# Windowed attention ahead of two expert layers: key spans copied unscaled, refills ahead of stores, one averaging group per head pair, and TensorE's stages one unit closer behind the scores

## The chip, the cores and the metric

The kernel runs on one core of one Trainium2 chip. The metric is the device time of one execution in microseconds. The kernel before has a median of 1250.22 us over 3 runs (1250.11 to 1251.17).

## The reference

The program computes an attention layer and two layers of experts. The change touches the attention alone; its core is

```
k_sum = k.reshape(B, H, nb, block, D).max(axis=3)
v_sum = v.reshape(B, H, nb, block, D).mean(axis=3)
scores_l = scale * np.matmul(q, k.transpose(0, 1, 3, 2))
mask_l = np.abs(pos[:, None] - pos[None, :]) < window
scores_s = scale * np.einsum('bhsd,bhnd->bhsn', q, k_sum)
scores_s = scores_s + np.log(block)
scores_l_m = np.where(mask_l, scores_l, -1000000000.0)
a = softmax over concatenate([scores_l_m, scores_s])
attn_out = np.matmul(a, np.concatenate([v, v_sum], axis=2))
```

with B = 4 batches, H = 8 heads, S = 768 positions, D = 64, block 32 (so 24 blocks), window 16 and scale 1/8. All is float32. The rows of the result then go through a first expert layer with a gate (argmax over logits, one of 8 experts) and a second with a capacity per expert, assigned in the order of the logits.

## The kernel before

**Tiling.** Two heads make a head pair, so each batch has 4 pairs and the program 16. A pair's 768 queries are worked off in 3 units of 256 queries; a batch has 12 units, the program 48. For 64 queries at a time the window touches a span of 96 keys, so one score matmul is 64 queries against 96 span keys and 24 block maxima, 120 columns. The tile `k_bias` (two buffers, by pair) holds these columns: span keys and maxima in partitions 0 to 63, mask and bias in partitions 64 to 127, met by an identity in the lower half of `q_eye`. So one matmul gives the masked scores.

**Who does what.** For each pair GpSimd (`key_spans`, L471 and L472) multiplies the raw keys `k_raw` by the scale into the 12 overlapping spans of both heads, four instructions. VectorE (`block_maxima`, L1017 and L1020) takes the block maxima of the raw keys in two halves and writes them, scaled, beside the spans. TensorE averages the values per block (`means`, L616), 12 matmuls of 64 columns for each of the two heads; VectorE takes them out of PSUM (L1029), and GpSimd spreads them into `va` (`spread_means`, L482).

**Units.** TensorE, ScalarE and VectorE each run one loop over units n = 0 to 47 and on. In iteration n TensorE does the scores of unit n (L597), the transposes of the probabilities of unit n-2 (L606), at two of three iterations one head of `means` for the next pair, the values of unit n-3 (L634), the transposes of the finished rows of unit n-4 (L648) and, for a batch's last three units, the gate's logits of unit n-5 (L657). ScalarE copies the transposed probabilities out (L867), then the transposed rows (L872), and then does the exponentials of unit n (L859). VectorE takes the maxima of the scores of unit n (L1054), the means, then normalises unit n-3 (L1061 to L1068), and then reduces block maxima of the next pair. The first 6 iterations (`LEAD`) stand ahead of a loop over the batches. After each batch's loop VectorE and ScalarE do the gate's decision (`route`), whose end is `x_ready`.

**Order of the work.** All of it is written by hand; each engine's queue is in order and semaphores join them. SyncE's queue issues all loads and stores of the attention, pair by pair: for pair hp it refills the keys and queries two pairs ahead (`refill_k`, `refill_q`), then the values of the next batch, which wait for `pv_done` of this pair, then stores the rows of pair hp-1. At hp = 0 that store is the last pair's of the batch before, and it waits for `x_ready`. Keys and queries have two buffers, the values four.

Of the kernel before, what the change touches and what calls it, by code (L numbers as in the profile page):

```python
# [15 lines left out]
P = 128  # L16
# [38 lines left out]
LEAD = 6  # L55
# [47 lines left out]
def two_layers_of_experts(nc, q, k, v_win, modality_id, w_gate, modality_bias, w1, w2,  # L103
                          w_gate2, w1b, w2b, out):
    ctx = ExitStack()
    with ctx:
# [57 lines left out]
        ksum_done = sem("ksum_done")  # L164
# [4 lines left out]
        scores_done = sem("scores_done")  # L169
        nmax_done = sem("nmax_done")  # L170
# [158 lines left out]
        def attention_steps(eng, unit, route=None):  # L329
# [5 lines left out]
            def element(b, own):  # L335
                for n in range(LEAD, UNITS + LEAD):
                    unit(b, n, own)
                if route:
                    route(b)
# [8 lines left out]
        def _(sp):  # L348
# [21 lines left out]
            with sp.Fori(0, B) as b:  # L370
                for hp in range(HP):
                    def refill_k(nb, nhp):
                        sp.wait_ge(spans_done, HP * b + hp + 1)
                        sp.wait_ge(ksum_done, HP * b + hp + 1)
                        load_k(nb, nhp)
# [25 lines left out]
                    else:  # L401
# [39 lines left out]
        def _(pool):  # L441
# [4 lines left out]
            pool.dma_start(mid[:, :, :], modality_id.bitcast(I32).rearrange("(j p t) -> p j t", p=P, t=2)).then_inc(modality_loaded, 16)  # L446
            for t in kraw:
                chain(g.memset(t[:, :, 0:WINDOW], 0.0))
                chain(g.memset(t[:, :, WINDOW + S:KW], 0.0))
            g.nop().then_inc(pads_ready, 1)  # L450
            chain(g.memset(ident[:, :], 0.0))
            chain(g.affine_select(out=ident[:, :], in_=ident[:, :], compare_op=ALU.not_equal, fill=1.0,
                                  base=0, pattern=[[-1, P]], channel_multiplier=1))
            g.nop().then_inc(eye_ready, 1)
            span = span_mask[D:P, 0:WK]
            chain(g.memset(span_mask[D:P, WK:PW], math.log(BLOCK)))
# [5 lines left out]
            g.nop().then_inc(mask_ready, 1)  # L462

            def key_spans(m):
# [3 lines left out]
                for h in range(2):  # L468
                    pieces = kraw[m % 2][:, h, 0:S].rearrange("d (j c) -> d j c", c=QB)
                    after = kraw[m % 2][:, h, QB:QB + S].rearrange("d (j c) -> d j c", c=QB)  # L470
                    g.tensor_scalar(kbt[m % 2][0:D, h, :, 0:QB], pieces, SCALE, None, ALU.mult).then_inc(pool_chain, 1)  # L471
                    last = g.tensor_scalar(kbt[m % 2][0:D, h, :, QB:WK], after[:, :, 0:WK - QB], SCALE, None, ALU.mult)  # L472
                    last.then_inc(pool_chain, 1)
                    chain.n += 2
                pool.wait_ge(pool_chain, chain.n)
                g.nop().then_inc(spans_done, 1)  # L476

            def spread_means(m):
                pool.wait_ge(means_taken, 2 * (m + 1))
# [5 lines left out]
            key_spans(0)  # L485
# [97 lines left out]
        def _(pe):  # L583
            mm, tr = nc.tensor.matmul, nc.tensor.transpose
            def scores(b, n):
                hp, i = n // PU, n % PU
                if i == 0:
                    pe.wait_ge(q_loaded[hp % 2], 16 * (HP // 2 * b + hp // 2 + 1))
                    pe.wait_ge(spans_done, HP * b + hp + 1)
                    pe.wait_ge(ksum_done, HP * b + hp + 1)  # L590
# [18 lines left out]
            def means(b, m, h, n):  # L609
                pe.wait_ge(vw_loaded[m % HP], 16 * (b + m // HP + 1))  # L610
                if m or h or not isinstance(b, int):
                    pe.wait_ge(means_taken, 2 * (HP * b + m) + h)
                if n >= 5:
                    pe.wait_ge(x_done, UNITS * b + n - 4)
                for j in range(NQ):
                    last = mm(bank[4 + (n + 1) % 2][WK:PW, MEAN0:MEAN0 + D], average[:, j, :], va[m % HP][0:WK, h, j, 0:D],  # L616
# [3 lines left out]
            def values(b, n):  # L620
# [7 lines left out]
                else:  # L628
                    pe.wait_ge(means_taken, 4)
# [31 lines left out]
            pe.wait_ge(const_ready, 1)  # L661
# [3 lines left out]
            def unit(b, n, own):  # L665

                own(scores, n, n)
                if n >= 2:
# [10 lines left out]
                if n >= 5:  # L679
                    own(first_logits, n - 5, n - 5)  # L680

            means(0, 0, 0, 0)
            means(0, 0, 1, 1)
# [161 lines left out]
        def _(act):  # L845
# [3 lines left out]
            for t in qe:  # L849
                last = nc.scalar.activation(t[D:P, :, :].rearrange("p h (j u) -> p (h j) u", u=QB),  # L850
                                            ident[D:P, D:P].unsqueeze(1).to_broadcast([P - D, 2 * NQ, QB]), ACT.Copy)
            last.then_inc(eye_rows, 1)

            def exponentials(b, n):
# [27 lines left out]
            def unit(b, n, own):  # L882

                if n >= 2:
                    own(copy_probs, n - 2, n - 2)
                if n >= 4:
                    own(copy_x, n - 4, n - 4)
                own(exponentials, n, n)
                if n >= 5:
                    own(copy_logits, n - 5, n - 5)  # L890
# [5 lines left out]
            attention_steps(act, unit, route)  # L896
# [101 lines left out]
        def _(dve):  # L998
# [4 lines left out]
            for t in kbt:  # L1003
# [4 lines left out]
            vec.nop().then_inc(bias_rows, 1)  # L1008

            def block_maxima(b, m, h):  # L1010

                if h == 0:
                    dve.wait_ge(k_loaded[m % 2], 16 * (HP // 2 * b + m // 2 + 1))
                    if m or not isinstance(b, int):
                        dve.wait_ge(ksum_done, HP * b + m)
                own_keys = kraw[m % 2][:, h, WINDOW:WINDOW + S].rearrange("p (n t) -> p n t", t=BLOCK)
                vec.tensor_reduce(ksum[:, h, :], own_keys, AXX, ALU.max).then_inc(bmax_done, 1)  # L1017
                if h == 1:
                    dve.wait_ge(bmax_done, 2 * (HP * b + m) + 2)
                    vec.tensor_scalar(kbt[m % 2][0:D, :, :, WK:PW], ksum[:, :, :].unsqueeze(2).to_broadcast([D, 2, NQ, NB]), SCALE, None, ALU.mult  # L1020
# [432 lines left out]
```

## Time and profile before

| | |
|---|---|
| median of 3 runs | 1250.22 us |
| the profiled execution | 1257.53 us |
| its span | 1255.8 us, mean granted clock 0.84 |
| first score matmul | 24.76 us from the span's start |
| scores of the last unit (47) | 257.43 us |
| first weights of the experts requested | 276.85 us |
| TensorE matmuls busy | 956.8 us (76%) |
| VectorE, ScalarE, GpSimd busy | 560.7, 325.4, 281.2 us |

Times in views are microseconds from the span's start. In a timeline a row is one instruction or a run of equal ones: start, duration, engine and line, what it writes and reads, and in square brackets how long the engine was idle before and what ended that. PE is TensorE's matmuls and PEld its weight loads, DVE is VectorE, ACT ScalarE, POOL GpSimd, SP SyncE; a q behind a name is that engine's queue. A float32 matmul shows as two records, so 8 matmuls are x16. The end of a matmul row is modelled, so the distance from one row's start to the next one's is what a stage takes.

### The profile page before, as it was taken

Reading aid. Unit: us, or ns where it says so; the run is one execution under the profiler, and the core shown is the slowest. Engines: PE = TensorE matmul, PEld = TensorE weight load, DVE = VectorE, ACT = ScalarE, POOL = GpSimd, SP = SyncE. Lnnn points to the kernel's source line nnn. Section 1 sums busy time; section 2 is a strip of 40 time slices with the busy share of each in tenths; the row PEclk is TensorE's granted clock in tenths of the full one; section 3 lists DMA queues with packets and bytes.
Section 4 is the critical chain, followed back from the end, with each engine's and each line's share of the span. In section 5 each row is a group of like instructions: output and inputs, shape, how many; then the busy total and the mean of one; then the engine's idle time right before and its main releaser. Section 6 shows DMA issues by size and latency. Waiting matters only on the chain.

```text
span 1255.8 us, 24355 instructions
## 1 busy us (share of the span) xinstructions
PE 956.8 (76%) x7844; PEld 792.0 (63%) x7845; DVE 560.7 (45%) x1581; ACT 325.4 (26%) x659; POOL 281.2 (22%) x324
## 2 busy tenths in 40 slices
PE   3898988872799999999994333333229999999995
PEld 3676777661588888888883222222227888888884
DVE  3645444547422222222223776667663434444431
ACT  2443434322322222222223000000004443443421
POOL 7755535501012111211111000000001222222220
PEclk9997878865899999999997555555559999999998
DMA  7565536424611111111112000000023343444310
GB/s 142 116 122 115 113 86 119 85 49 165 241 42 42 42 34 34 44 41 34 35 41 84 5 0 0 0 0 0 0 77 108 115 171 126 159 176 176 109 34 25
DMA packets 45988, 97.49 MB, mean 78 GB/s; under 512 B 7248, under 2 KB 19584, under 8 KB 45952
## 3 DMA queue, kind: packets, MB, share of 16 engines
q1 hardware_dynamic: 37888, 70.56, 20.9%
q0 software_dynamic: 8064, 26.46, 6.2%
q8 instruction: 21, 0.34, 0.1%
q14 instruction: 15, 0.12, 0.0%
HBM read 77.49 MB, written 19.51 MB: 77 GB/s over the span
## 4 chain that ended last, share of the span: by engine, by line
PE 59%; issue 24%; POOL 5%; DVE 5%; DMA 4%; ACT 1%; SPq 1%; DVEq 0%; ACTq 0%; POOLq 0%
PE bank L704 41%; DMA k_raw<-in_k 3%; PE bank L728 3%; PE bank L616 3%; PE bank L597 3%; POOL k_bias L471 3%; PE bank L711 2%; PE bank L657 2%; PE bank L751 2%; PE bank L606 1%; PE bank L634 1%; POOL k_bias L472 1%; PE bank L744 1%; PE bank L648 1%; DMA xg<-x_rows,gidx 1%
## 5 line engine op out<-in xcount | busy, mean ns | idle before, releaser
L704 PE MATMUL bank<-W,xh 128*128 (+1 forms) x784 | 254.8, 407 | 13.5 <-DVE gates L1202 10.6
L704 PE MATMUL bank<-W,hh 128*128 (+1 forms) x784 | 252.5, 403 | 10.2 <-DVE hl L1209 10.2
L704 PEld LDWEIGHTS bank<-W,xh 128*128 128x128 f32 x784 | 146.4, 192 | 46.3 <-issue 11.3
L704 PEld LDWEIGHTS bank<-W,hh 128*128 128x128 f32 x784 | 145.3, 190 | 42.5 <-issue 9.0
L704 PE MATMUL bank<-W,xl 128*128 (+1 forms) x392 | 156.5, 399 | 0.0
L704 PE MATMUL bank<-W,hl 128*128 (+1 forms) x392 | 156.0, 398 | 0.0
L795 PE MATMUL bank<-ge,cb 128*8 128x16 bf16 x1344 | 42.3, 172 | 106.5 <-DVE ge L1321 106.5
L538 POOL COPY sidx<-idx 128x1 int32 (+1 forms) x49 | 27.2, 556 | 366.9 <-DVE y L1217 247.7
L795 PEld LDWEIGHTS bank<-ge,cb 128*8 128x8 bf16 x1344 | 36.1, 83 | 111.8 <-DVE ge L1321 111.8
L1209 DVE TENSOR_TENSOR hl<-bank,hh 128x512 fp32r<-128x512 f32 x98 | 63.1, 686 | 95.9 <-ACT hh L898 91.7
L529 POOL COPY gidx<-idx 128x1 int32 (+1 forms) x50 | 10.6, 212 | 406.3 <-DVEq L1152 293.1
L898 ACT ACTIVATE xh<-bank 128x512 fp32r<-128x512 f32 x50 | 29.8, 595 | 269.5 <-PE bank L711 269.5
L1196 DVE TENSOR_TENSOR W<-raw_w,W 128x1024 f32 (+1 forms) x80 | 93.0, 1218 | 6.1 <-ACT W L898 5.9
L471 POOL TENSOR_SCALAR k_bias<-k_raw 64x768 f32<-64x768 f32 x32 | 70.2, 2195 | 92.5 <-DMA k_raw<-in_k 91.8
L898 ACT ACTIVATE hh<-bank 128x512 fp32r<-128x512 f32 x98 | 53.1, 597 | 137.1 <-PE bank L728 137.1
L704 PEld LDWEIGHTS bank<-W,xl 128*128 128x128 f32 x392 | 74.9, 191 | 18.2
L898 ACT ACTIVATE W<-raw_w 128x1024 f32 (+1 forms) x80 | 78.6, 1055 | 29.7 <-SPq L424 28.0
L704 PEld LDWEIGHTS bank<-W,hl 128*128 128x128 f32 x392 | 74.3, 190 | 17.8
L922 ACT ACTIVATE hid<-bank 128x512 f32<-128x512 f32 x98 | 59.1, 604 | 86.9 <-PE bank L704 86.9
L597 PE MATMUL bank<-k_bias,q_eye 128*64 128x120 f32 x768 | 59.1, 305 | 23.5 <-POOLq L476 21.4
L616 PE MATMUL bank<-va,average 96*24 96x64 f32 x768 | 59.1, 243 | 19.3 <-POOLq L496 18.9
L1200 DVE TENSOR_TENSOR xl<-bank,xh 128x512 fp32r<-128x512 f32 x50 | 34.6, 692 | 82.7 <-ACT xh L898 82.7
(234 smaller groups left out, 1289.5 us busy)
## 6 DMA issues: line engine op xcount, KB each, us to landing
raw_w<-in_moe_w SPq DMA_DIRECT2D x20, 2048.0 KB, 9.4
va<-in_v_win SPq DMA_DIRECT2D x16, 585.0 KB, 4.9
k_raw<-in_k SPq DMA_DIRECT2D x16, 384.0 KB, 8.1
q_eye<-in_q SPq DMA_DIRECT2D x16, 384.0 KB, 8.1
x_rows<-x SPq DMA_DIRECT2D x12, 384.0 KB, 9.2
x_rows<-x SPq DMA_DIRECT2D x4, 387.0 KB, 5.4
xg<-x_rows,gidx POOLq DMA_INDIRECT x26, 3.4
y_rows<-y,sidx POOLq DMA_INDIRECT x25, 2.8
```

Of the source, the lines that this page charges most:

```text
L471: g.tensor_scalar(kbt[m % 2][0:D, h, :, 0:QB], pieces, SCALE, None, ALU.mult).then_inc(pool_chain, 1)
L538: chain(g.tensor_copy(sidx[:, :], idx[:, bass.ds(val(i), 1)]))
L597: last = mm(bank[n % 2][QB * s_:QB * s_ + QB, PW * (2 * t + h):PW * (2 * t + h) + PW], qe[hp % 2][:, h, QB * j:QB * j + QB], kbt[hp % 2][: ...
L616: last = mm(bank[4 + (n + 1) % 2][WK:PW, MEAN0:MEAN0 + D], average[:, j, :], va[m % HP][0:WK, h, j, 0:D], start=j == 0, stop=j == NQ - 1)
L704: last = mm(ps, lhs[a][:, c, :], rhs[b](c), start=c == 0 and t == 0, stop=c == n - 1 and t == 2)
L728: last = tr(bank[2 + c // 4][:, P * (c % 4):P * (c % 4) + P], hid[:, P * c:P * c + P], ident[:, :])
L795: last = mm(bank[7][0:E, 0:KSEARCH], cb[:, j, :], ge[:, j, :], start=j == 0, stop=j == TC - 1)
L898: copy = lambda o, a: nc.scalar.activation(o, a, ACT.Copy)
L922: nc.scalar.activation(hid[:, 512 * half:512 * half + 512], bank[half][:, :], ACT.Relu).then_inc(relu_done[st], 1)
L1196: tt(o, r, hi.bitcast(F32), ALU.subtract).then_inc(wlo_done[st], 1)
L1200: ins = tt(xl[:, :, :].rearrange("p c t -> p (c t)"), bank[4][:, :], xh[:, :, :].rearrange("p c t -> p (c t)").bitcast(F32), ALU.subtract)
L1209: tt(hl[:, f, :].rearrange("p c t -> p (c t)"), bank[2 + half][:, :], hh[:, f, :].rearrange("p c t -> p (c t)").bitcast(F32), ALU.subtract ...
```

## The change

- `LEAD` is 5: TensorE does the transposes of the probabilities of unit n-1 in iteration n, values of unit n-2, transposed rows of n-3, logits of n-4; ScalarE and VectorE follow.
- GpSimd copies the keys into the spans unscaled, four `tensor_copy`, and in a fifth copies the block maxima, which VectorE wrote before; it waits for VectorE's two reductions. `ksum_done` is gone. The scale is applied after the scores: ScalarE's exponential gets `scale=SCALE`, and VectorE multiplies the 4 negated maxima of a unit by it, a new instruction of 128x4 behind a wait on the reduction. The bias of the block columns is divided by the scale.
- SyncE's store that waits for `x_ready` stands at hp = 1, behind that pair's refills and its other store.
- `means` of a pair is one group of 12 matmuls of 128 columns (both heads), in every third iteration, and VectorE takes it out in one copy.
- At the start GpSimd's span mask comes first and the load of the modality last; VectorE builds the spans of the first pair (`first_spans`); TensorE does the first scores ahead of the first means.
- `route` is cut in two: its first three VectorE instructions follow the iteration in which the last logits come.

```diff
-LEAD = 6
+LEAD = 5
...
-                    else:
+                    if hp == 1:
                         with sp.If(b > 0):
                             sp.wait_ge(x_ready, b)
...
-                    g.tensor_scalar(kbt[m % 2][0:D, h, :, 0:QB], pieces, SCALE, None, ALU.mult).then_inc(pool_chain, 1)
-                    last = g.tensor_scalar(kbt[m % 2][0:D, h, :, QB:WK], after[:, :, 0:WK - QB], SCALE, None, ALU.mult)
...
+                    chain(g.tensor_copy(kbt[m % 2][0:D, h, :, 0:QB], pieces))
+                    chain(g.tensor_copy(kbt[m % 2][0:D, h, :, QB:WK], later[:, :, 0:WK - QB]))
+                pool.wait_ge(bmax_done, 2 * (m + 1))
+                chain(g.tensor_copy(kbt[m % 2][0:D, :, :, WK:PW], ksum[:, :, :].unsqueeze(2).to_broadcast([D, 2, NQ, NB])))
                 g.nop().then_inc(spans_done, 1)
...
-                if n >= 2:
-                    own(transpose_probs, n - 2, n - 2)
-                if n % PU < 2:
-                    m = n // PU + 1
-                    own(means, PU * m, m, n % PU, n)
-                if n >= 3:
-                    own(values, n - 3, n - 3)
-                if n >= 4:
-                    own(transpose_rows, n - 4, n - 4)
...
+                if n >= 1:
+                    own(transpose_probs, n - 1, n - 1)
...
+                if n % PU == 1:
+                    m = n // PU + 1
+                    own(means, PU * m, m, n)
+                if n >= 2:
+                    own(values, n - 2, n - 2)
+                if n >= 3:
+                    own(transpose_rows, n - 3, n - 3)
...
-                                                bias=nmax[n % 2][:, a:a + 1])
+                                                bias=nmax[n % 2][:, a:a + 1], scale=SCALE)
...
-                                  AXX, ALU.max, negate=True).then_inc(nmax_done, 1)
+                                  AXX, ALU.max, negate=True).then_inc(max_done, 1)
+                dve.wait_ge(max_done, UNITS * b + n + 1)
+                vec.tensor_scalar(nmax[n % 2][:, :], nmax[n % 2][:, :], SCALE, None, ALU.mult).then_inc(nmax_done, 1)
```

TensorE's queue, iteration 7 of the first batch. Of the buffer numbers, a unit's scores are in bank 0 or 1, its transposed probabilities in bank 2 or 3, its values in bank 4 or 5 and its rows in bank 6 or 7, by the unit's parity; `probs` goes round three buffers. Before:

```order
L597 MATMUL bank1<-k_bias0,q_eye0 64x120 x8
L606 MATMUL bank3<-ident,probs2 120x128 x4
L612 REGISTER_ALU
L616 MATMUL bank4<-va3,average 24x64 x12
L634 MATMUL bank4<-va1,pt0 64x65 x8
L648 MATMUL bank7<-ident,x 128x128 x2
```

and of the changed kernel:

```order
L596 MATMUL bank1<-k_bias0,q_eye0 64x120 x8
L601 REGISTER_ALU
L605 MATMUL bank2<-ident,probs0 120x128 x4
L609 ISA
L615 MATMUL bank5<-va3,average 24x128 x12
L633 MATMUL bank5<-va1,pt1 64x65 x8
L647 MATMUL bank6<-ident,x 128x128 x2
```

The stages stand in the same order, but behind the scores of unit 7 the transposes now read `probs0`, the exponentials of unit 6, where they read `probs2`, those of unit 5. ScalarE's queue for iteration 6 reads before

```order
L867 ACTIVATE pt0<-bank2 120x512
L872 ACTIVATE xt<-bank6 128x256
L855 REGISTER_ALU
L857 REGISTER_ALU
L859 ACTIVATE probs0<-bank0,nmax0 128x120 x4
```

and of the changed kernel

```order
L864 REGISTER_ALU
L865 ACTIVATE pt1<-bank3 120x512
L870 ACTIVATE xt<-bank7 128x256
L853 REGISTER_ALU
L857 ACTIVATE probs0<-bank0,nmax0 128x120 x4
```

The copies belong to units 5 and 3 now, before to 4 and 2; the exponentials of unit 6 still stand behind the copy of the transposed rows, which TensorE makes last in its iteration 6. In SyncE's queue the store that waits for `x_ready` (129 columns wide) moves like this:

```order
-L402 COMPARE_AND_BRANCH
-L396 ISA
-L396 DMA x_rows<-x 128x6x129
-L402 UNCONDITIONAL_BRANCH
+L387 UNCONDITIONAL_BRANCH
 L373 REGISTER_ALU
 L353 ISA
 L353 DMA k_raw<-in_k 64x2x768
```

The load of the keys of a batch's last pair no longer stands behind it; the store now comes one pair later, ahead of the load of the next batch's first keys.

## Rows read from the trace of the kernel before

**Rows 1.** The chain that ended last, 24.8 to 276.8 us, by line:
```profile
by line: DMA k_raw<-in_k 16.6%; PE bank L597 13.3%; PE bank L616 12.4%; POOL k_bias L471 10.0%; PE bank L657 8.5%; PE bank L606 7.2%; PE bank L634 7.1%; POOL k_bias L472 5.4%; issue 3.8%; PE bank L648 3.5%; SPq L396 1.2%; DVE ksum L1017 1.1
```
**Rows 2.** Busy time by stretch: length; PE, PEld, DVE, ACT, POOL; granted clock; DMA share, GB/s:
```profile
71.70:132.50 60.80, 54.26 (x698) 45.79 (x698) 30.76 (x76) 23.88 (x72) 33.49 (x21) 0.86 0.56 114
132.50:202.70 70.20, 61.86 (x698) 52.65 (x698) 30.62 (x80) 24.77 (x76) 31.82 (x20) 0.76 0.51 101
...
276.80:1255.80 979.00, 732.62 (x5060) 602.13 (x5060) 430.17 (x1252) 222.05 (x351) 139.44 (x198) 0.83 0.21 70
32.00:34.00 2.00, 1.19 (x19) 0.87 (x17) 1.49 (x2) 1.05 (x3) 1.60 (x4) 1.00 0.46 104
```
**Rows 3.** Pieces of that chain in order of time: start, duration, what:
```profile
55.59 9.41 DMA k_raw<-in_k
...
70.43 1.15 POOL k_bias L472
71.74 1.87 PE bank L597 x16
...
83.72 1.69 PE bank L657 x16
...
150.16 2.69 PE bank L616 x24
```
**Rows 4.** Who waited for whom, 0 to 210 us: total, times, longest:
```profile
POOL k_bias L471 <- DMA k_raw<-in_k: 67.4, 10, 16.4
```
**Rows 5.** Timeline, one iteration with `means` at the full clock:
```profile
77.11 1.04 PE L597 MATMUL bank<-k_bias,q_eye 128*64 128x120 f32 x16
...
78.08 0.65 PE L606 MATMUL bank<-ident,probs 128*120 128x128 f32 x4
...
78.66 1.53 PE L616 MATMUL bank<-va,average 96*24 96x64 f32 x24
...
80.12 0.69 PE L634 MATMUL bank<-va,pt 120*64 120x65 f32 x16
...
80.74 0.44 PE L648 MATMUL bank<-ident,x 128*128 128x128 f32 x2
...
81.11 1.04 PE L597 MATMUL bank<-k_bias,q_eye 128*64 128x120 f32 x16
...
81.22 0.39 ACT L872 ACTIVATE xt<-bank 128x256 f32<-128x256 f32 x1 [1.85 <-PE bank L648]
...
81.50 1.11 ACT L859 ACTIVATE probs<-bank,nmax 128x120 f32<-128x120 f32 x4
...
81.92 0.93 DVE L1017 TENSOR_REDUCE ksum<-k_raw 64x24 f32<-64x768 f32 x1
```
**Rows 6.** GpSimd's groups by form: busy, mean ns of one | idle before, releaser:
```profile
L471 POOL TENSOR_SCALAR k_bias<-k_raw 64x768 f32<-64x768 f32 x32 | 70.2, 2195 | 92.5 <-DMA k_raw<-in_k 91.8 <-POOL iota_e L510 0.3 <-POOL span_mask L460 0.2
...
L482 POOL COPY va<-vst 24x1536 f32<-24x1536 f32 x16 | 23.4, 1465 | 11.3 <-DVE vst L1029 8.2 <-POOL k_bias L472 3.1
```
**Rows 7.** Timeline of the start and of two later places:
```profile
6.50 4.40 POOL L471 TENSOR_SCALAR k_bias<-k_raw 64x768 f32<-64x768 f32 x1 [0.21 <-POOL span_mask L460]
...
33.08 1.04 PE L597 MATMUL bank<-k_bias,q_eye 128*64 128x120 f32 x16 [0.81 <-DVE k_bias L1020]
...
43.00 1.43 DVE L1041 CAST midf<-mid 128x24 f32<-128x24 int32 x1
...
99.15 0.35 SPq L357 DMA_DIRECT2D va<-in_v_win  x1
...
104.07 0.43 SPq L396 DMA_DIRECT2D x_rows<-x  x1
...
257.43 1.04 PE L597 MATMUL bank<-k_bias,q_eye 128*64 128x120 f32 x16
```
**Rows 8.** DMA issues: KB each, median us to landing (first: the load issued at 8.75):
```profile
va<-in_v_win SPq DMA_DIRECT2D x1, 585.0 KB, 9.7
```
**Rows 9.** The same view over the whole span:
```profile
k_raw<-in_k SPq DMA_DIRECT2D x16, 384.0 KB, 8.1
```

More of the change, by code:

```diff
@@ L337, in element @@
                     unit(b, n, own)
-                if route:
-                    route(b)
+                    if route and n in route:
+                        route[n](b)
             with eng.Fori(0, B - 1) as b:
@@ L445, in _ @@
                 pool.sem_inc(stored, 16)
[L446 to L454, printed above, removed]
             span = span_mask[D:P, 0:WK]
-            chain(g.memset(span_mask[D:P, WK:PW], math.log(BLOCK)))
+            chain(g.memset(span_mask[D:P, WK:PW], math.log(BLOCK) / SCALE))
             chain(g.memset(span, 0.0))
@@ L462, in _ @@
             g.nop().then_inc(mask_ready, 1)
+            chain(g.memset(ident[:, :], 0.0))
+            chain(g.affine_select(out=ident[:, :], in_=ident[:, :], compare_op=ALU.not_equal, fill=1.0,
+                                  base=0, pattern=[[-1, P]], channel_multiplier=1))
+            g.nop().then_inc(eye_ready, 1)
+            for t in kraw:
+                chain(g.memset(t[:, :, 0:WINDOW], 0.0))
+                chain(g.memset(t[:, :, WINDOW + S:KW], 0.0))
+            g.nop().then_inc(pads_ready, 1)
+            pool.dma_start(mid[:, :, :], modality_id.bitcast(I32).rearrange("(j p t) -> p j t", p=P, t=2)).then_inc(modality_loaded, 16)
             def key_spans(m):
@@ L607, in transpose_probs, with means @@
                 last.then_inc(pt_done, 1)
-            def means(b, m, h, n):
+            def means(b, m, n):
                 pe.wait_ge(vw_loaded[m % HP], 16 * (b + m // HP + 1))
[L611 to L614, printed above, removed]
+                if m or not isinstance(b, int):
+                    pe.wait_ge(means_taken, HP * b + m)
+                if n >= 4:
+                    pe.wait_ge(x_done, UNITS * b + n - 3)
                 for j in range(NQ):
-                    last = mm(bank[4 + (n + 1) % 2][WK:PW, MEAN0:MEAN0 + D], average[:, j, :], va[m % HP][0:WK, h, j, 0:D],
+                    last = mm(bank[4 + n % 2][WK:PW, MEAN0:MEAN0 + 2 * D], average[:, j, :], va[m % HP][0:WK, :, j, 0:D],
                               start=j == 0, stop=j == NQ - 1)
@@ L882, in unit @@
             def unit(b, n, own):
-                if n >= 2:
-                    own(copy_probs, n - 2, n - 2)
+                if n >= 1:
+                    own(copy_probs, n - 1, n - 1)
+                if n >= 3:
+                    own(copy_x, n - 3, n - 3)
+                own(exponentials, n, n)
                 if n >= 4:
[L887 to L890, printed above, removed]
+                    own(copy_logits, n - 4, n - 4)
             def route(b):
@@ L894, in route @@
                 nc.scalar.activation(lexp[:, :, :], lsh[:, :, :], ACT.Exp).then_inc(route_exp_out, 1)
-            attention_steps(act, unit, route)
+            attention_steps(act, unit, {UNITS + LEAD - 1: route})
             copy = lambda o, a: nc.scalar.activation(o, a, ACT.Copy)
@@ L1083, in unit, with route_shift @@
                     token_biases()
[L1085 removed]
+            def route_shift(b):
                 chain.start(pre + per * b)
@@ L1103, in route @@
                 assert chain.n == per, (chain.n, per)
-            attention_steps(dve, unit, route)
+            attention_steps(dve, unit, {UNITS + LEAD - 2: route_shift, UNITS + LEAD - 1: route})
             tt, ts, stt, red = vec.tensor_tensor, vec.tensor_scalar, vec.scalar_tensor_tensor, vec.tensor_reduce
```

80 lines of the change are left out of this document (43 added, 37 removed).

## The prediction, made before the changed kernel ran

> **What bounds the kernel now.** I read the chain of waits first. Over the whole span the experts' matmuls lead it, and nothing of them changes, so the question is the attention, 24.8 to 276.8 us. There the chain is not TensorE alone: 16.6% of it is the load of the keys, 15.4% GpSimd's making of the spans out of them [rows 1]. The busy table by stretch says the same from the other side: in 60.8 us, the second batch's length, TensorE works 54.3 us at a granted clock of 0.86, in the third batch, 70.2 us long, 61.9 us at 0.76 [rows 2]. So it loses both ways, by standing and by the low clock afterwards. The chain in order of time shows one such stand: keys asked for at 55.59 land 9.41 us later, GpSimd's last span ends at 71.58, and the scores start at 71.74 in 1.87 us instead of 1.04 [rows 3, 5]. GpSimd waited 67.4 us in 10 such places [rows 4].
>
> The timeline at the full clock gives what TensorE needs. From one start to the next: scores 0.97, transposes 0.58, one head of means 1.46, values 0.62, transposed rows 0.37, together 4.00 [rows 5]; without means 2.54; the gate's logits add 1.69 [rows 3].
>
> **The change, part by part.** I count in iterations, with t(n) the start of the scores of unit n.
>
> *Keys.* The next load of keys goes out 1.3 us after the values of a pair's last unit. Those come one iteration earlier now, so the keys of a pair have the whole of four iterations less 1.3 us: from t(3p-4)+1.3 to t(3p). Landing takes 8.1 us in the median and 9.41 in the example [rows 3, 9]. GpSimd's multiplies take 2195 ns for 768 elements, 2.86 ns each; its only plain copy takes 1465 ns for 1536, 0.95 ns each [rows 6]. At the copy's rate the four copies cost 2 x (0.73+0.37) plus starts, about 2.9 us instead of 6.6, and the fifth, of the maxima, 0.64. The bounds are a copy like the copy (3.5 us in all) and a copy like the multiply (6.6 + 1.6 = 8.2 us). I take the first, since it is the same operation, though on 24 partitions there and 64 here.
>
> The GPSIMD Engine Reference of the Trainium skill (section 3.1, on elementwise cycle accounting) speaks against this: it gives one rate, about a cycle per element, for bodies of at most two operations, so a multiply by a constant and a copy would cost the same and the copies would bring nothing. The rows disagree, 2.86 ns against 0.95 [rows 6]; by the page's rule this would be the case of slow copies below, 1280.
>
> So keys landing at t(3p-4)+9.4 to 10.7 are spans by +14.2 at the latest. Four iterations are 15.4 (below). The second half of the maxima is made behind the normalising of the iteration before t(3p-1) and ends 1.74 us into an iteration (81.92+0.93-81.11) [rows 5]; with the fifth copy the spans are ready about 2.7 us into one that lasts 3.1. The load is hidden, narrowly.
>
> *The exponentials.* Here the closer stages cost. ScalarE does the exponentials of unit n behind the copy of transposed rows that TensorE makes last in its iteration n, before as after. They start at t(n+1)+0.39 and end at +1.50 (81.50+1.11-81.11) [rows 5]. Before, their transposes came two iterations later. Now they come at t(n+1)+0.97, so TensorE waits until about +1.57: 0.6 us in every iteration, unless logits stand between (three of twelve). A plain iteration is then 3.14, one with means 0.6 above its work.
>
> *Means.* 12 matmuls of 128 columns replace 24 of 64. The 24 records of 64 columns take 1.46 us at the full clock and 2.69 at the low one [rows 3, 5], 61 and 112 ns each, so they follow the array's clock, and 64 columns at two cycles are 53 ns of the 61. With 128 I take 115 ns, 2.75 us a group against 2.92 for both before. The bounds: 61 ns (1.46 us) if the 61 were fixed, and 145 ns (0.58/4, transposes of 128 columns) [rows 5], 3.48 us.
>
> *Route.* SyncE issued the values at 99.15 and the store behind `x_ready` at 104.07 [rows 7]: 4.9 us for the keys behind it, three times; gone. In its place the two stores at hp = 1 put 384 KB more ahead of the next keys in one iteration of two batches; at the 185 GB/s that 1.74 MB in 9.41 us make, 2.1 us, of which about 1.5 shows, since VectorE's block maxima stand in its queue ahead of the maxima of the scores. The second half of `route` holds the maxima of unit 5 to about 4.8 us into its iteration, where the exponentials would start at 3.5: 1.2 us a batch.
>
> *A batch.* 8 plain iterations of 2.54, 4 with means of 5.29, three logits of 1.69, nine waits of 0.6, 1.2 for route: 20.3+21.2+5.1+5.4+1.2 = 53.2 us. Before, the second and third batch took 60.8 and 70.2 [rows 2], and all three after the first 62.9 on average (257.43-71.74, and one iteration of 3.1) [rows 3, 7].
>
> *Small edits.* The 128x4 multiply on VectorE, some 0.25 us a unit, lies before exponentials that wait for TensorE anyhow; if that cover goes it is 0.25 a unit, 12 us in all. The scale in the activation I take as free, since its activations already carry a bias.
>
> *Start.* The first scores no longer stand behind GpSimd's first spans, but the values of unit 0 need both first means and the second pair's maxima: the values of pair 1 land at 8.75+9.7 = 18.45 [rows 8], its means take some 4 us while the clock is low, then 0.23+0.94 on VectorE and 0.64+1.47 on GpSimd, about 25.9, so scores of unit 3 at about 27 instead of 33.08 [rows 7]. VectorE's wide copies slow GpSimd at the start (4.40 us for a multiply of 2.2) [rows 6, 7]; the same load hides that. From unit 3 to 12: six plain 3.14, three with means 5.9, and 2.0 for the modality's instructions on VectorE (from 43.00 on) [rows 7]: 38.6, so unit 12 at 65.6 instead of 71.74.
>
> *Sum.* The scores of unit 47: 65.6 + 3 x 53.2 - 3.14 = 222.1, plus 3.0 for the two double stores. Six gaps of 2 to 3 us stay (modality, three routes, two double stores); each may bring the low clock for a few stages (2.69 for 1.46), 1.5 us each, 9 in all. So 234.1 instead of 257.43 [rows 7]: 23.3 earlier. The drain behind it is one iteration shorter, 2.0. Together 25.3. The 979 us behind it [rows 2] only move. The profiled execution took 1257.5, 7.3 above the median, so it would be 1232, and the median 1250.2-25.3 = 1225.
>
> **Rivals.**
> *Means cheap*: 61 ns a record. For it: scores of 120 columns also show 0.97 us for 16, 61 each. Against: those alternate between two halves of the array's columns and can overlap. 16 x 1.29 = 21 us more gained: 1204.
> *Keys still late*: the loads are packed into 12.2 us a pair instead of 15.5, and if they land after 10.7 or more, VectorE's block maxima hold everything behind them. Nine pairs at about 1.2 and nearly as much for the clock: some 17 us given back, 1242. For it: 9.41 [rows 3] is not rare; against: the DMA share is only 0.51 to 0.56 [rows 2].
> *GpSimd copies as slowly as it multiplies* (slower than before): 8.2 us from landing to spans, so scores 18.9 us after t(3p-4), 3.5 late. It decides from about 4.8 us on. Three pairs a batch give 3 x (3.5+2.5 for the clock) = 18 us; with 53.2 that is 71.2 against 62.9 before, 25 over three batches, and two such pairs in the first put unit 12 at 77.6, 6 late. About 30 slower: 1280.
> *The small waits bring the low clock down for good*: TensorE waits 0.6 us in three of four iterations. For it: after a stand of 2 us at 71.74 the scores went at the low clock [rows 3]. At that clock the stages take 1.85 times as long (2.69 for 1.46), some 86 us a batch instead of 53: about 1355. The Trainium skill has such a case ("TensorE: Matmul & The Clock Gate", section on a second HAM failure mode): an engine that idles briefly between groups can fall back and recover over and over. Against it: from 32 to 34 us TensorE worked 1.19 of 2.0 us and was granted 1.00 [rows 2].
>
> **How the numbers follow.** The forecast (keys hidden, exponentials set the pace) has 0.60, its own range 1214 to 1236. Means cheap 0.14, keys late 0.16, slow copies 0.05, low clock 0.03, the rest 0.02. The range reaches from 1203, the cheap means, to 1242, the late keys; outside lie the two slower cases and tails. A measurement of this kernel tells a change from none at about 0.2%, 2.5 us. Faster by more: all but the slow cases and a tail of the late keys, 0.91; within it 0.02; slower 0.07.
>
> **What would show it.** Right: scores to scores about 3.1 us in plain iterations, each with TensorE released by ScalarE's exponentials; GpSimd copies of 0.7 to 0.9 us; a means group of 2.7 to 2.8; keys landed before VectorE's queue reaches them; clock near 1 between 70 and 230. Wrong: plain iterations of 2.5 (the exponentials did not wait), GpSimd releasing TensorE at pair starts (keys or copies late), a means group of 1.5, or the expert stages changing their length.

## The result: slower where faster was forecast, and the profile after

The changed kernel takes 1261.86 us (median of 4 runs, 1258.05 to 1267.49); the kernel before took 1250.26 beside it (4 runs). The ratio is 1.0091, with a 95% interval of 1.0055 to 1.0127: 0.9% slower, and 37 us over the forecast of 1225. The profiled executions are 1259.62 (span 1257.4) and 1257.53 (span 1255.8), only 2 us apart, because the profiled execution of before was a long one for that kernel.

The experts' stage has kept its length: 978.63 us behind the first request for weights, which went out at 278.77 (979.00 behind 276.8 before [rows 2]). So it is again the attention alone. Its chain by line from the first scores (10.94) on:

```profile
by line: DMA k_raw<-in_k 20.4%; PE bank L615 13.2%; PE bank L605 9.1%; PE bank L633 8.9%; PE bank L656 7.5%; ACT probs L857 7.2%; PE bank L596 6.4%; issue 5.9%; PE bank L647 4.4%; DVE nmax L1061 2.0%; DVE ksum L1016 1.8%; DVE oh L326 1.8%; 
```

GpSimd's spans, 15.4% of the chain before [rows 1], are gone from it, as was meant. The keys have not gone: 20.4% where 16.6% stood. The busy table by stretch (length; PE, PEld, DVE, ACT, POOL; granted clock; DMA share, GB/s) has the second and third batch first, and then two stretches inside the second:

```profile
68.37:137.66 69.29, 51.27 (x600) 41.72 (x600) 32.61 (x85) 24.65 (x76) 19.96 (x25) 0.87 0.69 115
137.66:202.85 65.19, 50.90 (x601) 41.47 (x600) 32.37 (x84) 24.72 (x76) 19.08 (x25) 0.89 0.65 107
...
120.00:125.00 5.00, 4.49 (x58) 3.66 (x55) 0.00 (x0) 0.82 (x2) 0.00 (x0) 1.00 1.29 95
278.77:1257.40 978.63, 732.81 (x5060) 602.44 (x5060) 430.18 (x1252) 222.02 (x351) 139.17 (x198) 0.83 0.21 70
```

A batch takes 69.3 and 65.2 us where 53.2 was forecast. TensorE's work did shrink (51 busy us for 54.3 and 61.9), and its clock is no worse than before (0.87 and 0.89 for 0.86 and 0.76 [rows 2]); it stands 18 and 14 us a batch. And there is something odd from 120 to 125 us: the DMA engines are counted busier than in any stretch of [rows 2] (1.29; the packets' times overlap), yet they move 95 GB/s, less than the 114 at a share of 0.56 in [rows 2]. What lies there is a pair of stores. From the timeline and the chain of that place:

```profile
111.27 0.33 SPq L357 DMA_DIRECT2D va<-in_v_win  x1
111.79 1.15 SPq L395 DMA_DIRECT2D x_rows<-x  x2
113.28 0.95 SPq L353 DMA_DIRECT2D k_raw<-in_k  x1
...
131.42 0.94 DVE L1016 TENSOR_REDUCE ksum<-k_raw 64x24 f32<-64x768 f32 x1 [13.24 <-DMA k_raw<-in_k]
...
133.77 1.11 ACT L857 ACTIVATE probs<-bank,nmax 128x120 f32<-128x120 f32 x4 [9.83 <-DVE nmax L1064]
...
134.94 1.11 PE L605 MATMUL bank<-ident,probs 128*120 128x128 f32 x4 [10.45 <-ACT probs L857]
```

```profile
113.28 18.11 DMA k_raw<-in_k
181.22 15.38 DMA k_raw<-in_k
```

The keys asked for right behind the two stores land after 18.11 us, against 9.41 in [rows 3]. VectorE's block maxima wait for them with the maxima of the scores behind them in the queue, so ScalarE gets no maxima and TensorE no probabilities: it stands 10.45 us, although the scores whose probabilities it waits for (unit 22, at 117.60) were made before and need none of the late keys. The iteration from unit 23 to 24 takes 14.2 us instead of 3.1, the one a batch later (35 to 36) 11.5. The issue view over the span says the same of medians (KB each, us to landing):

```profile
k_raw<-in_k SPq DMA_DIRECT2D x16, 384.0 KB, 9.9
...
x_rows<-x SPq DMA_DIRECT2D x12, 384.0 KB, 10.8
x_rows<-x SPq DMA_DIRECT2D x4, 387.0 KB, 12.5
```

The keys took 8.1 before [rows 9]; the store of 387 KB, which now stands behind another, is the slowest of all.

The second new gap is at the gate's decision, once a batch; the timeline from unit 17 on:

```profile
94.11 1.04 PE L596 MATMUL bank<-k_bias,q_eye 128*64 128x120 f32 x16
...
96.95 1.47 POOL L480 COPY va<-vst 24x1536 f32<-24x1536 f32 x1 [0.23 <-POOL k_bias L473]
97.15 1.49 DVE L326 TENSOR_TENSOR oh<-iota_e,lidx 128x48 f32 x1
97.30 1.04 PE L596 MATMUL bank<-k_bias,q_eye 128*64 128x120 f32 x16
...
100.27 0.66 DVE L1061 TENSOR_REDUCE nmax<-bank 128x4 f32<-128x480 f32 x1 [0.76 <-DVE x L1115]
...
101.63 1.11 ACT L857 ACTIVATE probs<-bank,nmax 128x120 f32<-128x120 f32 x4 [3.84 <-DVE nmax L1064]
...
102.80 1.11 PE L605 MATMUL bank<-ident,probs 128*120 128x128 f32 x4 [4.46 <-ACT probs L857]
```

The scores of unit 17 start at 94.11 and those of unit 18 at 97.30. The maxima of unit 17 start only at 100.27, behind the second half of `route`, and its exponentials at 101.63, so TensorE stands 4.46 us ahead of its transposes in iteration 18 and then goes at the lower clock (transposes in 1.11 us instead of 0.65). These three iterations take 8.2, 7.5 and 8.3 us instead of 3.1.

What came as forecast is in these rows, a plain iteration (unit 46 to 47), the groups of GpSimd and `means` (busy, mean ns of one | idle before), and the list of waits:

```profile
253.84 0.65 PE L605 MATMUL bank<-ident,probs 128*120 128x128 f32 x4 [0.51 <-ACT probs L857]
254.42 0.69 PE L633 MATMUL bank<-va,pt 120*64 120x65 f32 x16
255.03 0.44 PE L647 MATMUL bank<-ident,x 128*128 128x128 f32 x2
255.40 1.04 PE L596 MATMUL bank<-k_bias,q_eye 128*64 128x120 f32 x16
```

```profile
L615 PE MATMUL bank<-va,average 96*24 96x128 f32 x384 | 47.2, 280 | 0.6 <-POOLq L493 0.6
...
L470 POOL COPY k_bias<-k_raw 64x768 f32<-64x768 f32 x30 | 24.6, 820 | 69.1 <-DMA k_raw<-in_k 67.3 <-POOL va L480 0.5 <-POOL iota_e L507 0.2
...
L471 POOL COPY k_bias<-k_raw 64x384 f32<-64x384 f32 x30 | 15.1, 502 | 1.8
```

```profile
POOL k_bias L473 <- DVE ksum L1016: 81.7, 15, 12.8
POOL k_bias L470 <- DMA k_raw<-in_k: 67.3, 10, 15.7
...
PE bank L605 <- ACT probs L857: 48.2, 31, 10.4
```

In iteration 46 TensorE waits 0.51 us for the exponentials and the iteration is 3.1 us long; the copies take 820 ns instead of the 2195 of [rows 6]. The records of L615 overlap, so their mean is no length; from start to start a group of 24 takes 2.73 us (90.40 to 93.13).

### The profile page after: what moved, and what is told of

Same layout as the page of the kernel before. It is cut to its first block, busy times and chain, and to the rows that moved or that the text cites. A ratio compares the mean times of both kernels' runs of the same rounds, so it can differ in the third digit from the quotient of the medians.

```text
span 1257.4 us, 23551 instructions
## 1 busy us (share of the span) xinstructions
PE 945.7 (75%) x7460; PEld 776.0 (62%) x7461; DVE 568.1 (45%) x1602; ACT 325.4 (26%) x659; POOL 227.9 (18%) x335
## 4 chain that ended last, share of the span: by engine, by line
PE 59%; issue 25%; DVE 5%; DMA 5%; ACT 2%; POOL 2%; SPq 1%; DVEq 0%; ACTq 0%; POOLq 0%
PE bank L703 41%; DMA k_raw<-in_k 4%; PE bank L727 3%; PE bank L615 3%; PE bank L605 2%; PE bank L633 2%; PE bank L710 2%; PE bank L656 2%; PE bank L750 2%; ACT probs L857 2%; PE bank L596 1%; PE bank L647 1%; PE bank L743 1%; ACT W L896 1%; DMA xg<-x_rows,gidx 0%
## 5 line engine op out<-in xcount | busy, mean ns | idle before, releaser
L703 PE MATMUL bank<-W,xh 128*128 (+1 forms) x784 | 254.6, 406 | 13.4 <-DVE gates L1216 10.5
L703 PEld LDWEIGHTS bank<-W,xl 128*128 128x128 f32 x392 | 74.9, 191 | 18.1
L605 PE MATMUL bank<-ident,probs 128*120 128x128 f32 x192 | 36.4, 320 | 48.2 <-ACT probs L857 48.2
L896 ACT ACTIVATE yt<-bank 128x512 f32<-128x512 f32 x25 | 14.9, 597 | 217.7 <-PE bank L743 217.7
L1239 DVE TENSOR_SCALAR y<-bank,gates 128x512 f32<-128x512 f32 x25 | 18.8, 751 | 114.6 <-PE bank L703 114.6
```

The costliest lines, as they stand in the source:

```text
L605: last = tr(bank[2 + n % 2][0:PW, P * a:P * a + P], probs[n % 3][:, a, :], ident[:, :])
L703: last = mm(ps, lhs[a][:, c, :], rhs[b](c), start=c == 0 and t == 0, stop=c == n - 1 and t == 2)
L896: copy = lambda o, a: nc.scalar.activation(o, a, ACT.Copy)
```

## The experiments

Theory: the two stores together make the keys late, and that is most of the loss; `route` on VectorE is the rest. Rivals: the volume ahead of the keys (then the shape of rows is indifferent); the refills ahead of the store as such (then separating the two stores at the same hp brings nothing); the copies or the closer stages themselves cost the time. Each run's ratio is to runs of the kernel before on its own chip. "Start of the experts" is the first request for weights, 276.85 before and 278.77 after.

**1. The store back at hp = 0.** In the changed kernel:

```diff
-                    if hp == 1:
+                    if hp == 0:
                         with sp.If(b > 0):
                             sp.wait_ge(x_ready, b)
```

> The changed kernel with one edit undone: the store of a batch's last pair stands at hp = 0 again, where the kernel before had it, alone behind that pair's refills. Theory A (two stores of x_rows in flight at once slow each other and everything queued with them; in the changed kernel keys landed after 18.1 and 15.4 us behind the double store, where they took 8 to 10 elsewhere): no landing of keys above 11 us, rows of 516 bytes at about 32 ns a packet instead of 129, and the time falls by 10 to 18 us, to about 1246. Theory B (the transfers are simply packed closer because every stage is faster): landings of 12 us and more stay, and the time stays within 3 us of the changed kernel's, since the keys now also wait some 5 us for x_ready three times.

Measured: 1238.34 us, ratio 0.990 [0.985, 0.995]. Start of the experts 257.48. The keys' median landing is 8.0 and none after the first three takes over 9.7:

```profile
k_raw<-in_k SPq DMA_DIRECT2D x16, 384.0 KB, 8.0
...
x_rows<-x SPq DMA_DIRECT2D x4, 387.0 KB, 5.5
```

So the placing of one store decides the sign of the whole change: some 24 us, more than the 10 to 18 expected, although the wait for `x_ready` (a store issued 5.8 us behind the values) is back with it.

**2. The move alone.** In the kernel before:

```diff
-                    else:
+                    if hp == 1:
                         with sp.If(b > 0):
                             sp.wait_ge(x_ready, b)
```

> The kernel before with that one edit alone: the store that waits for x_ready moved to hp = 1. Theory A: the two stores meet here too, keys behind them land after 13 us or more twice, and the kernel is 5 to 20 us slower than before. Theory B: the three waits of 4.9 us are gone and no landing grows beyond 11 us: 5 to 12 us faster than before.

Measured: 1247.93 (10 runs), ratio 0.9985 [0.996, 1.001]: no change, so neither of the two times expected came, but the late landings did. The waits for `x_ready` are gone; its chain has

```profile
115.89 16.27 DMA k_raw<-in_k
```

and the iterations at these places take 16.3 and 11.6 us. The slow landing belongs to the move, not to the stages or the copies. That the kernel before pays for it with what the same move gains, and the changed kernel with its closer stages does not, is a reading that no run separates.

**3. Both stores at hp = 1, but apart.** In the changed kernel, the `x_ready` store goes between the queries' refill and the next values:

```diff
                         refill_q(b, hp + 2)
+                    if hp == 1:
+                        with sp.If(b > 0):
+                            sp.wait_ge(x_ready, b)
+                            store_x(..., HP - 1)
                     with sp.If(b < B - 1):
...
                         store_x(b, hp - 1)
-                    if hp == 1:
...
```

> The changed kernel with the store that waits for x_ready at hp = 1 but ahead of that pair's refill of values, so that about 8 us and the values' load lie between the two stores. Theory A: the landings above 13 us go, packets of 516 bytes fall from 129 ns to under 50, and the time falls by 10 to 20 us, to 1242 to 1252. Theory B: as many bytes in as short a stretch, so landings stay and the time is within 3 us of the changed kernel's.

Measured: 1237.22 (7 runs), ratio 0.9904 [0.9875, 0.9933]. Start of the experts 258.04. The store goes out at 97.29, the pair's own at 110.01, and the keys behind it land in 9.31 us:

```profile
97.29 0.43 SPq L386 DMA_DIRECT2D x_rows<-x  x1
...
110.01 0.41 SPq L386 DMA_DIRECT2D x_rows<-x  x1
110.77 0.58 SPq L353 DMA_DIRECT2D k_raw<-in_k  x1
```

```profile
110.77 9.31 DMA k_raw<-in_k
```

The refills ahead of the store were no fault; the wide store (129 columns) right behind the narrow one (128) was. The iteration from unit 23 to 24 is 3.7 us. The experiment changes two things at once, the distance of the two stores and their order: the wide one now goes first. The last batch has no values to refill, so there the same two stores go out 0.81 us apart, wide first. They land as they do alone (5.0 and 9.9 us in the batch shown above), and the wide one's packets take 28.7 ns:

```profile
213.39 1.18 SPq L386 DMA_DIRECT2D x_rows<-x  x2
...
x_rows<-x SPq DMA_DIRECT2D x1, 387.0 KB, 5.4
x_rows<-x SPq DMA_DIRECT2D x1, 384.0 KB, 9.9
```

So closeness alone is not the fault. Whether the order decides or how far the two really overlap, no run tests.

**4. Rows padded, the stores still together.** The rows of `x_rows` are 513 floats, 2052 bytes, apart, so their pieces of 512 bytes begin at any multiple of 4 bytes. Here they are 2112 bytes apart; the last store is 144 columns wide. VectorE fills them and the gathers' tile `xg` is as wide, two edits not shown:

```diff
-XW = DM + 1
+XW = DM + 16
...
-                        cols = slice(P * shp, P * shp + P + (shp == HP - 1))
+                        cols = slice(P * shp, P * shp + P + 16 * (shp == HP - 1))
```

> The changed kernel with rows of x_rows 528 floats apart (2112 bytes, a multiple of 64) instead of 513 (2052 bytes); the last pair's store is then 144 columns wide, 576 bytes a row, and the double store stays. Theory A with misaligned rows as the cause of the slowness: the wide packets fall from 129 ns to about 35, the landings to 10 or 11 us, and the time by 10 to 18 us. Theory A with the mere overlap of two stores as the cause: wide packets stay near 129 ns and the time within 4 us of the changed kernel's. The gathers of the first expert layer get 3% more bytes, which should not show.

Measured: 1237.34, ratio 0.989 [0.983, 0.995]. Start of the experts 259.78; their stage is no shorter (981.0 us). Landings are shorter than in any kernel so far, with more bytes in each fourth store:

```profile
k_raw<-in_k SPq DMA_DIRECT2D x16, 384.0 KB, 6.7
...
x_rows<-x SPq DMA_DIRECT2D x4, 432.0 KB, 4.9
```

That excludes the volume. The rival of the double store's bytes, which is also how the prediction priced it, falls.

**5. The kernel before with padded rows** tells whether the pitch matters where stores are single. It is before with the edit of experiment 4.

> The kernel before with its rows padded to 2112 bytes (144 columns in the last of the four stores instead of 129); its two stores are never in flight together. If misaligned rows cost only where two stores overlap, as the short packets of 31.5 ns in the kernel before and 34.2 ns in the changed kernel with its stores apart suggest, the time is that of the kernel before, 0.995 to 1.003 of it, and the 512-byte packets fall from 50.9 ns to about 31 without anyone waiting for them. If misaligned rows cost in every store, the keys behind the stores land 1 to 2 us earlier and the ratio is 0.985 to 0.993.

Measured: 1250.26 (10 runs), ratio 0.999 [0.996, 1.002], the same; yet the keys land in 6.7 us (median) instead of 8.1, and the one that took 9.41 [rows 3] now takes 6.7. The first half of the expectation holds for the time, the second for the landings: single stores are slowed by the pitch too, but before the change nobody collects those 2.7 us. The records of the packets put the kernels side by side: mean ns of one packet of the narrow stores (512 bytes, all twelve) and of the wide ones (516 or 576 bytes, the first three; the fourth goes out alone behind the last batch, at 32 to 35 ns everywhere):

```
kernel                       row pitch  stores    512 B   516 or 576 B
before                       2052 B     single     50.9     31.5
after                        2052 B     double     58.3    129.0
2, move alone                2052 B     double     52.9     99.4
1, store back                2052 B     single     50.5     31.3
3, apart                     2052 B     single     53.0     34.7
4, padded                    2112 B     double     31.0     33.8
5, before padded             2112 B     single     30.4     31.5
```

It takes both, the odd pitch and a wide store right behind a narrow one, to make a packet of 516 bytes take 99 to 129 ns instead of 31 to 35. "Single" is not quite that in the last batch: the kernel before issues a wide store at 235.87 and a narrow one at 238.24, before the first has landed, and experiment 3 the two above; in both the wide one goes first and its packets take 31.8 and 28.7 ns. Why the other order is slow (two writers in one piece of memory, or something else) no run here shows.

**6. `route` one iteration earlier.** Experiment 3 with the second half of `route` moved up to the first, in both queues:

```diff
-            attention_steps(act, unit, {UNITS + LEAD - 1: route})
+            attention_steps(act, unit, {UNITS + LEAD - 2: route})
...
-            attention_steps(dve, unit, {UNITS + LEAD - 2: route_shift, UNITS + LEAD - 1: route})
+            attention_steps(dve, unit, {UNITS + LEAD - 2: lambda b: (route_shift(b), route(b))})
```

> The version with the stores apart, and the whole of route, on ScalarE and VectorE, one iteration earlier, ahead of the iteration with means that TensorE works 5.3 us on. Theory A (route stands in VectorE's queue ahead of the maxima of unit 5 and costs its iteration 4 to 5 us: 8.2, 7.7 and 8.2 us instead of 3.1, and about 0.8 in the one behind): 12 to 17 us faster, the three iterations 3.1 to 4 us. Theory B (the delay only moves, since route now stands ahead of the maxima of unit 4): the iteration of unit 4 grows from 5.3 to 8 us or more and the time stays within 4 us.

Measured: 1224.80, ratio 0.9778 [0.972, 0.984]. Start of the experts 243.97, 14.1 us earlier than in experiment 3. The iterations that took 8.2, 7.7 and 8.2 us in experiment 3 take 3.1, 3.0 and 3.1, since the iteration in which the decision now lies, one with `means` (5.3 us), is long enough to cover it:

```profile
90.72 0.38 DVE L326 TENSOR_TENSOR oh<-iota_e,lidx 128x48 f32 x1
...
92.65 0.66 DVE L1061 TENSOR_REDUCE nmax<-bank 128x4 f32<-128x480 f32 x1 [0.67 <-DVE x L1115]
```

**7. The same edit with the stores together**, that is the changed kernel with the edit of experiment 6, asks whether the two losses add.

> The changed kernel with the whole of route one iteration earlier on ScalarE and VectorE, and the two stores still together at hp = 1. If the two losses, double store and route, are separate and add, this stands as far below the changed kernel as the same edit did with the stores apart (12 to 16 us): 1246 to 1250, 0.996 to 1.000 of the kernel before. If most of route's delay lies beside the late keys, it brings under 6 us: 1256 to 1261, 1.004 to 1.009.

Measured: 1241.75 (9 runs), ratio 0.9939 [0.991, 0.997]. Against 1.0091 that is 1.5%, some 19 us (the two come from different chips, and the two intervals leave 13 to 25), at or above the 12 to 16 expected. They add, as far as these intervals tell.

**8. The spans multiplied again.** Experiment 3 with the four copies as multiplies by 1.0:

```diff
-                    chain(g.tensor_copy(kbt[m % 2][0:D, h, :, 0:QB], pieces))
+                    chain(g.tensor_scalar(kbt[m % 2][0:D, h, :, 0:QB], pieces, 1.0, None, ALU.mult))
```

> The version with the stores apart, and GpSimd making the four span pieces with a multiply by 1.0 instead of a copy (same values). It prices the copies. Theory A (the copies are a third as long and lie on the path from keys to scores): multiplies of 2.1 and 1.2 us, 4 us more from landing to spans, scores late by 2 us or more at most pairs and the low clock behind it: 15 to 30 us slower than with the copies. Theory B (the landing and VectorE's maxima cover them): within 4 us.

Measured: 1248.36 (10 runs), ratio 0.9963 [0.994, 0.999], so the copies are worth 0.6% or 7 us in this setting, between the two cases expected. Start of the experts 267.54 against 258.04.

```profile
L470 POOL TENSOR_SCALAR k_bias<-k_raw 64x768 f32<-64x768 f32 x30 | 63.7, 2124 | 48.7 <-DMA k_raw<-in_k 39.7 <-PE bank L596 6.9 <-POOL iota_e L507 0.3
```

The same bytes in the same shape: 2124 ns by a multiply, 820 by a copy. The case of slow copies had the direction right and, at some 30 us, was too dear: from unit 23 to 24 it takes 6.1 us instead of 3.7 and the iteration behind it 4.5 instead of 2.9, so 3.9 at this pair, where 6 were counted at each.

**9. Exponentials ahead of the copy of the rows.** Experiment 3 with ScalarE's two last steps exchanged:

```diff
+                own(exponentials, n, n)
...
-                own(exponentials, n, n)
```

> The version with the stores apart (1237 us), and on ScalarE the exponentials of unit n now ahead of the copy of the transposed rows of unit n-3. Theory A (that order makes TensorE wait 0.5 us in nine of twelve iterations, the price of the closer stages): plain iterations fall from 3.1 to 2.5 or 2.7 us, the sum of TensorE's waits for the exponentials from 37.6 to under 15 us, and the time by 8 to 16 us; not by the full 18, since four iterations then last 12.9 us and keys need about 13.3. Theory B (something else, such as the spans at 2.7 us into an iteration or VectorE's work, stands right behind): plain iterations stay at 3.0 or more and the time within 4 us.

Measured: 1232.54, ratio 0.984 [0.978, 0.990], some 8 us under experiment 3 by the ratios, whose intervals overlap. The wait of 0.51 us is gone and plain iterations take 2.7 instead of 3.1 us, but the second and third batch take 58.5 and 57.8 us, as in experiment 3 (58.0 and 57.6), and unit 47 starts at 235.07 instead of 234.67. What the stages save comes back as waits for the keys (from unit 23 to 24 6.0 us instead of 3.7) and at `route` (8.8 instead of 8.2). Only the drain, the stretch behind the last unit's scores, keeps it: start of the experts 17.6 us behind unit 47 instead of 23.4.

**10. All of it:** stores apart, rows padded, exponentials first, `route` early.

> Stores apart, rows of x_rows 2112 bytes apart, exponentials first and route early, together. If each part's gain stands by itself: 1237 less 8 to 16, less 12 to 17, less some 2 for faster landings, so 1202 to 1217. If the transfers of the keys become the bound (1.74 MB a pair in 9 us at best, against iterations that give 10.6 us a pair): waits for the keys come back and the time stays above 1217.

Measured: 1204.05, ratio 0.9638 [0.957, 0.971], 3.6% under the kernel before and the fastest of all. Start of the experts 219.10. Its second and third batch:

```profile
64.85:112.39 47.54, 46.87 (x601) 38.62 (x601) 31.31 (x83) 24.29 (x77) 19.06 (x24) 1.00 0.63 151
112.39:159.91 47.52, 46.86 (x600) 38.60 (x600) 31.70 (x83) 24.27 (x77) 19.07 (x24) 1.00 0.64 152
```

TensorE is busy 46.9 of 47.5 us and is granted 1.00 throughout. Now the padding and the exchange on ScalarE pay: together they bring another 1.4% over experiment 6 (0.5 to 2.3 by the intervals), where the padding changed nothing for the kernel before, and the exchange left the batches as long as they were.

## Why the prediction was wrong

The forecast was 1225 and the time 1261.9. The sum had 1.5 us for the low clock behind each of the two double stores and the three decisions, and those are counted with them here. By the ratios, each taken of 1250, the 37 us are:

| step of the prediction | forecast | measured | missed |
|---|---|---|---|
| two double stores, 3.0 and 3.0 for the clock | 6.0 | after less experiment 3: 0.0187 of 1250 = 23.4 | 17.4 |
| `route`, 1.2 a batch and 4.5 for the clock | 8.1 | experiment 3 less 6: 0.0126 = 15.8 | 7.7 |
| all the rest, gained: 25.3 + 6.0 + 8.1 | 39.4 | 1 less experiment 6: 0.0222 = 27.7 | 11.7 |

The runs come from different chips and each ratio has an interval of 0.3 to 0.6% to either side, so a row is good to some 6 to 8 us. The base (5.4) and the drain (6.0), both below, come to the 11.7 of the last row.

**The double store** is the step that failed. The prediction saw it ("the two stores at hp = 1 put 384 KB more ahead of the next keys") and priced it by bytes over a mean rate, 2.1 us, of which 1.5 shows. It measured 18.1 and 15.4 us of landing where 9.3 is usual, and 11 and 8 us more in the iteration that waits. The error was to take the queue as a pipe of constant rate. In the trace of before these two stores go out 9.6 us apart (104.07 and 113.69), or 2.4 with the wide one first (235.87 and 238.24), and the first lands in 5.4, so it had no row for a wide store right behind a narrow one. The step had one answer, without the two bounds given elsewhere; at the least the far end should have stood beside it, as a rival that ends slower. The rival "keys still late" has the right mechanism (block maxima hold everything behind them) with another cause, and at 1242 it was too cheap.

**`route`** had its mechanism right and its size wrong: 1.2 us a batch against 4.4 to 5.2 in the three iterations. The prediction let the maxima of the next scores come "about 4.8 us into" the iteration. In the trace they start 6.16 us into it (94.11 to 100.27), their scaling ends at 101.60, 7.5 us in, and TensorE then starts at the lower clock. 1.1 us of the 7.5 is one instruction, `oh`, 1.49 us long instead of the 0.38 it takes in experiment 6. It lies beside GpSimd's copy from 96.95 to 98.42, and ends at 98.64.

**The base.** The sum was made against a profiled execution of 1257.5 us and its 25.3 taken off a median of 1250.2. But that execution is 7.3 us over the median, and its third batch took 70.2 us [rows 2]; in experiment 5, the same kernel but for the padding and the same in time, the profiled execution took 1250.84 and its third batch 62.7. So the surplus lies most likely in that batch, in the waits for keys that the change removes. A gain summed against a long execution is too large for a typical one. Experiment 6 shows it: its span is 33.1 us below that of before (1222.7 to 1255.8), its median only some 27.7, so 5.4 of the miss.

**The drain** was to be 2.0 us shorter; from unit 47 to the weights it takes 23.4 us instead of 19.4, so 6.0 were missed. The exponentials of the last units wait for nothing but their own place behind the rows' copy, TensorE stands 1.48 us and then goes at the lower clock. With the exponentials first it takes 17.6.

**Right** were: the plain iteration (3.14 forecast, 3.1) and its wait (0.6, measured 0.51); `means` at 2.73 for 2.75, so not the cheap case; the copies at 0.82 and 0.50 us for 0.73 and 0.37; unit 3 at 26.84 for 27; the keys all but hidden where no double store is in front (3.7 us from unit 23 to 24 in experiment 3, 3.1 in experiment 4). Without the two mis-sized terms the sum up to the last unit holds: a batch of 53.2 less 1.2 for `route` is 52.0, and in experiment 6 the batches take 53.6 and 52.2; unit 47 would be at 234.1 less 3.0, 3.6 and 7.5 for the clock, 220.0, and is at 220.62. The low clock did not take over: 0.87 and 0.89.

The multiply by the scale, "some 0.25 us a unit" beside other work, is mostly that, but not always. Beside GpSimd's copies it takes up to 0.86 us. Its line's instructions (ns, min/median/max), and two neighbours in a timeline:

```profile
L1064 DVE TENSOR_SCALAR nmax<-nmax x48: 170/171/861, 13.8 to 257.2; 128x4 f32<-128x4 f32 x48
```

```profile
73.92 0.82 POOL L470 COPY k_bias<-k_raw 64x768 f32<-64x768 f32 x1
74.00 0.77 DVE L1064 TENSOR_SCALAR nmax<-nmax 128x4 f32<-128x4 f32 x1
```

The multiply ends at 74.77, GpSimd's copy at 74.74. In the place at 131 us it is the same: the multiply from 132.97 ends at 133.74, the copy from 132.89 at 133.71. The Trainium skill says why ("SBUF — State Buffer", section "SBUF: two separate sides"): GpSimd and some instructions of VectorE, those with two SBUF inputs among them, share a pair of ports under an exclusive lock, and the later one waits for the whole of the other's instruction. `oh`, with two inputs, and the scaling, from SBUF to SBUF, behave so. The maxima of the scores, which read PSUM, do not (0.66 us at 100.27 ahead of the copies, 0.64 at 132.29 beside one), nor do those of the keys, which read one input in SBUF (0.94 at 131.42 beside the copy from 131.45). The multiply that the unscaled copies ask of VectorE therefore costs more beside them than the prediction counted.

**Open:** what in the memory or the DMA engines makes a wide store right behind a narrow one slow at the odd pitch, and whether the order or the distance decides; how much of experiment 10's last 1.4% is the padding and how much the exchange.

## What to carry to other kernels

Before a store is moved in a queue, look for what it will be in flight with, and do not price it by bytes over a mean rate: where the trace has no two such transfers together, put a bound far above it and try the move alone. Count a stage's engine queue to the end of the instruction that releases the next engine, with each instruction that ran longer beside one of GpSimd's at the length of GpSimd's. And do not take a gain that is summed against one profiled execution off the median: where that execution ran long, its surplus can be the very wait that goes.

## What the runs showed of the hardware that was not expected

- Stores of 512 and 516 bytes a packet to rows 2052 bytes apart: 51 and 31 ns a packet alone, 58 and 129 with the wide store 0.74 us behind a narrow one (wide first, 0.81 us apart in experiment 3, 28.7 for the wide); at 2112 bytes 31 and 34, together or not. The first loads of keys behind them land in 15.4 to 18.1 us in the changed kernel (13.4 to 16.3 in experiment 2), in 9.3 behind stores apart, and in 6.7 to 7.6 with padded rows.
- GpSimd's copy of 64x768 float32 takes 820 ns, its multiply by a constant 2124 (experiment 8) to 2195 [rows 6], on the same tiles.
- A 128x4 multiply on VectorE takes 171 ns, and up to 861 beside a GpSimd copy; it ends within 0.03 us of the copy's end in both places shown.
